# Gates ahead of x on VectorE, o products in pairs, and batch 0's root spread by TensorE, in a fused attention and two-MLP kernel

## The chip, the cores and the metric

One core of a Trainium2 chip runs the whole program. The metric is the device time of one execution in microseconds; the median of three runs of the kernel before is 894.88 us (893.85 to 895.17). TensorE's clock has two levels, 1.2 and 2.4 GHz, and the profile gives the granted one as a share of the higher.

## The reference

Three stages over batch 8, sequence 576, everything in float32:

```
kv  = einsum('bhsd,bhse->bhde', k, v)                    # 8 heads, d = 64
o   = einsum('bhsd,bhde->bhse', q, kv)
x   = o / sqrt(mean(o*o, -1) + 1e-6) * g_norm            # -> (8, 576, 512)

h   = relu(x @ w_in); u, v = h[..., :512], h[..., 512:]
v_n = (v - mean(v)) / sqrt(var(v) + 1e-6)                # over the last axis
gated = u * (einsum('ts,bsd->btd', w_spatial, v_n) + b_spatial[None, :, None])
y   = gated @ w_out

h   = relu(y @ w_in2)                                    # 512 -> 1024
c   = 3-tap convolution of h along the sequence
out = (h * sigmoid(c)) @ w_out2                          # 1024 -> 512
```

## The kernel before

**Numbers.** Large products take float32r operands, each split in a high part (a rounding copy on ScalarE) and a low part (value minus high part, a subtraction); three matmuls (high x high, high x low, low x high) make one product. `w_out @ w_in2` is multiplied once in the prologue into W (`w_product0` for its first half, `w_product` for its second), so the second stage writes only `gated`, through DRAM.

**Stages.** A prologue, up to 61.5 us; a body for each of the 8 batches, up to about 490 us (batches 1 to 6 in a loop, `body`; batch 0 written by itself in `first_body`; the last without work for a next batch); then `body2` for each batch of the third stage.

**The body of batch b** also makes x of batch b+1. On TensorE: k-v product of b+1 (80 matmuls); five v products (four of 128 rows with 12 matmuls of 512 columns, one of the last 64 rows with 8), and between them the four o products of b+1 and the sums of squares, one for each o; four u products (24 matmuls of 288 columns each); four spatial products (28 each). PSUM has eight banks: pairs 0, 1 and 2 (banks 0 to 5) take the u products in the order 0, 1, 2, 0 and the spatial ones in 1, 2, 0, 1; k-v uses bank 5, the sums of squares 4 and 5, o 6 and 7. So the fourth spatial product writes over the first, and waits for the gate that reads it (`s_g`, line 444); the k-v product of the next body waits for two gates (line 452), its v products for three and four (lines 404, 406) and for all four low parts of x (`s_x`, line 399).

**VectorE** (`body`, line 959) runs in this order: a copy of k-v; for each v tile statistics, the low part of the tile before, and normalising; the mean square; the last low part; `inverse_root` (five operations on 128x288); four `x_scale` (o times g times the spread root); four `gate` (spatial PSUM times u). **ScalarE**: relu of v, o_copy, square, high parts, roots, relu of u, and high parts of x (`x_hi`). **GpSimd** makes the low parts of x (`x_lo`, line 292) and the 64 left rows (`x_rows_left`).

**The root r** is in 4 x 4 rows after the sums of squares and must be on 64 partitions per head. `spread_r` on SP writes it to DRAM (4 DMAs), waits, and reads it back broadcast (2 DMAs) into `r_spread`; `x_scale` waits for that. Behind it on SP's queue stand the stores of the gated tiles; ahead of it the loads of k, v and q of batch b+2.

**The prologue.** SP loads two pieces of w_out and w_in2, then k, v, q of batch 0, then the other two pieces and the rest of w_in2, and once w_out is used, the second half of w_in; after the spread of batch 0's root the first half. TensorE: eight weight products, k-v of batch 0, its o products and sums of squares among further weight products, then the four `w_product`, each of which waits for its low part on VectorE (`W_lo`); then the body of batch 0, whose k-v product of batch 1 stands behind two v products. The low parts of the second half of w_in2, of w_in and w_spatial, and x's tiles 0 and 1 are on GpSimd.

## Time and profile before

| | us |
|---|---|
| median of 3 runs | 894.88 |
| profiled execution | 894.39 |
| its span | 892.6 |
| TensorE busy (matmul) | 841.5 (94%) |
| VectorE busy | 456.3 (51%) |
| ScalarE busy | 383.9 (43%) |
| GpSimd busy | 100.5 (11%) |
| mean granted clock | 0.962 |

The profile is of one execution. Busy times are shares of the span, averaged over stages that differ; matmuls are pipelined and their ends are modelled, so that the starts of successive groups give a better length than their busy time. A wait is put down to the semaphore that came last. The chain of waits is followed back from the last instruction. Times of windows and timelines count from the span's start.

### The profile page before, as it was taken

What the parts mean: (1) busy time and instruction counts of PE and PEld (TensorE: products, weight loads), DVE (VectorE), ACT (ScalarE), POOL (GpSimd) and SP (SyncE); (2) the same over time, 40 slices, a digit from 0 to 9 for tenths busy, and PEclk for the clock granted to TensorE, in tenths of its full rate; (3) what the DMA queues carried; (4) which work ended last, traced back from release to release, by engine and by line L of the source; (5) the groups of instructions that cost most, each with busy time, mean ns of one, the idle gap of its engine ahead of it and who ended that gap; (6) DMA issues with size and microseconds to landing.
All of it is one profiled execution on the core that took longest, in us unless ns stands there. A gap on an engine that the chain in (4) does not pass through costs nothing.

```text
span 892.6 us, 15537 instructions
## 1 busy us (share of the span) xinstructions
PE 841.5 (94%) x6038; PEld 743.9 (83%) x6038; DVE 456.3 (51%) x903; ACT 383.9 (43%) x666; POOL 100.5 (11%) x89
## 2 busy tenths in 40 slices
PE   6779799899998989989899999999999999999998
PEld 5456788878788787977889989899998989899996
DVE  2647356364463644536463746528281746538280
ACT  3426234152341533325133746537372736446371
POOL 1453030300203011030305000000000000000000
PEclk9879899899898998989999999999999999999999
DMA  8184341342413424231311101020201102020101
GB/s 301 48 293 143 105 160 55 94 171 54 159 54 109 155 54 159 80 114 60 93 67 44 65 36 66 34 80 1 101 1 57 56 35 65 35 76 0 47 0 59
DMA packets 24869, 75.49 MB, mean 85 GB/s; under 512 B 2434, under 2 KB 2690, under 8 KB 20740
## 3 DMA queue, kind: packets, MB, share of 16 engines
q1 hardware_dynamic: 24692, 75.04, 25.8%
q8 instruction: 21, 0.34, 0.2%
q14 instruction: 12, 0.10, 0.0%
q10 hardware_dynamic: 144, 0.01, 0.0%
HBM read 56.02 MB, written 19.02 MB: 84 GB/s over the span
## 4 chain that ended last, share of the span: by engine, by line
PE 70%; DVE 12%; DMA 7%; issue 5%; ACT 4%; SPq 1%; DVEq 0%; ACTq 0%
PE ps L393 32%; PE ps L566 22%; PE ps L422 9%; DMA r_spread<-r_scratch 5%; PE ps L355 2%; DVE o_x L911 2%; PE ps L372 2%; DVE r L897 2%; DMA kv_raw<-kv_rest_dram 1%; PE ps L508 1%; DMA r_scratch<-r 1%; DVE bn_stats L924 1%; ACT o_x L624 1%; PE ps L385 1%; DVE v_hg_split L950 1%
## 5 line engine op out<-in xcount | busy, mean ns | idle before, releaser
L393 PE MATMUL ps<-x_gated_split,w_product_split 128*128 128x288 f32 x1536 | 204.8, 294 | 0.0
L393 PEld LDWEIGHTS ps<-x_gated_split,w_product_split 128*128 128x128 f32 x1536 | 204.3, 188 | 0.5
L566 PE MATMUL ps<-w_in_split,v_hg_split 128*128 128x512 f32 x832 | 194.6, 389 | 0.0
L566 PEld LDWEIGHTS ps<-w_in_split,v_hg_split 128*128 128x128 f32 x832 | 155.7, 188 | 32.0
L393 PE MATMUL ps<-w_sp_split,v_hg_split 128*128 128x288 f32 x896 | 136.3, 317 | 21.3 <-DVE work L957 21.3
L393 PEld LDWEIGHTS ps<-w_sp_split,v_hg_split 128*128 128x128 f32 x896 | 133.8, 209 | 22.9 <-DVE work L957 22.9
L1053 DVE SCALAR_TENSOR_TENSOR work<-work,const_cols 128x576 f32<-128x576 f32 x64 | 52.4, 819 | 151.6 <-ACT work L815 151.6
L393 PE MATMUL ps<-x_gated_split,w_in_split 128*128 128x288 f32 x768 | 106.1, 298 | 1.1 <-DVE ms L890 0.6
L393 PEld LDWEIGHTS ps<-x_gated_split,w_in_split 128*128 128x128 f32 x768 | 103.7, 190 | 3.8 <-issue 1.8
L422 PE MATMUL ps<-w_in_split,x_gated_split 128*128 128x512 f32 x384 | 97.8, 406 | 6.1 <-issue 6.1
L422 PEld LDWEIGHTS ps<-w_in_split,x_gated_split 128*128 128x128 f32 x384 | 71.7, 192 | 27.2 <-issue 12.3
L292 POOL TENSOR_TENSOR x_gated_split<-o_x,x_gated_split 128x576 fp32r<-128x576 f32 x30 | 49.7, 1685 | 312.5 <-ACT x_gated_split L639 312.5
L810 ACT ACTIVATE work<-ps 128x576 f32<-128x576 f32 x64 | 41.8, 654 | 71.1 <-PE ps L393 59.7
L911 DVE SCALAR_TENSOR_TENSOR o_x<-o_x,const_cols,r_spread 128x576 f32<-128x576 f32 x32 | 33.2, 1101 | 74.6 <-DMA r_spread<-r_scratch 74.6
L846 ACT ACTIVATE o_x<-ps 128x512 f32<-128x512 f32 x32 | 19.1, 598 | 85.0 <-PE ps L566 85.0
L639 ACT ACTIVATE x_gated_split<-o_x 128x576 fp32r<-128x576 f32 x32 | 21.9, 684 | 78.3 <-DVE o_x L911 77.5
L1059 DVE SCALAR_TENSOR_TENSOR work<-work,const_cols 128x576 f32<-128x576 f32 x64 | 52.0, 813 | 0.6
L815 ACT ACTIVATE work<-work,const_cols 128x576 f32<-128x576 f32 x64 | 49.9, 779 | 2.1
L1064 DVE TENSOR_TENSOR work<-work 128x576 f32<-128x576 f32 x64 | 48.1, 751 | 0.3 <-ACT work L820 0.3
L957 DVE TENSOR_TENSOR work<-ps,work 128x576 f32<-128x576 f32 x32 | 22.8, 747 | 47.5 <-PE ps L393 47.5
L924 DVE BATCH_NORM_STATS2 bn_stats<-work 128x6 f32<-128x512 f32 (+1 forms) x40 | 27.7, 692 | 35.0 <-ACT work L651 28.8
L1070 DVE TENSOR_TENSOR v_hg_split<-work,v_hg_split 128x512 fp32r<-128x512 f32 x64 | 43.8, 685 | 0.0
(92 smaller groups left out, 729.1 us busy)
## 6 DMA issues: line engine op xcount, KB each, us to landing
kv_raw<-kv_main_dram SPq DMA_DIRECT2D x8, 2048.0 KB, 8.7
q_raw<-q_T_dram SPq DMA_DIRECT2D x8, 1152.0 KB, 5.1
r_spread<-r_scratch SPq DMA_DIRECT2D x16, 576.0 KB, 6.6
gated_scratch<-work SPq DMA_DIRECT2D x32, 288.0 KB, 2.2
q_raw<-gated_scratch SPq DMA_DIRECT2D x8, 1152.0 KB, 5.7
out_dram<-o_x SPq DMA_DIRECT2D x32, 256.0 KB, 2.0
work<-w_in_dram SPq DMA_DIRECT2D x3, 1024.0 KB, 9.3
kv_raw<-kv_rest_dram SPq DMA_DIRECT2D x8, 256.0 KB, 9.4
```

Of the source, the lines that this page charges most:

```text
L292: pool.tensor_tensor(XG[:, LO, m, :], o_T[:, m, :], XG[:, HI, m, :].bitcast(F32), ALU.subtract).then_inc(s_x, 1)
L393: last = pe.matmul(pair[bank][:, c, :], st, mo[:, c * HALF:(c + 1) * HALF], start=(n == 0), stop=(n == len(steps) - 1))
L422: last = pe.matmul(dst, x, w, start=(n == 0), stop=(n == len(st) - 1))
L566: last = pe.matmul(PS[:, ROW_BANK[i], :], x, wout2[:, w, f, :], start=(f == 0 and n == 0), stop=(f == FT - 1 and n == len(PASSES) - 1))
L810: act.activation(whole(h_sb[f % 3][:, 1:S + 1]), pair[f % 3], ACT.Relu).then_inc(s_hr, 1)
L815: act.activation(t_sb[f % 2], h_sb[f % 3][:, 1:S + 1], ACT.Copy, scale=cols[:, FT + f:FT + f + 1]).then_inc(s_t0, 1)
L911: dve.scalar_tensor_tensor(out=o_T[:, m, :], in0=o_T[:, m, :], scalar=g_col, in1=rB[:, m, :], op0=ALU.mult, op1=ALU.mult).then_inc(s_xm, 1)
L924: dve.bn_stats(stats[0:n, :], v_sb[i % 2][0:n, :]).then_inc(s_vst, 1)
L1053: dve.scalar_tensor_tensor(out=t, in0=h[:, 0:S], scalar=cols[:, f:f + 1], in1=t, op0=ALU.mult, op1=ALU.add).then_inc(s_cv1, 1)
L1059: dve.scalar_tensor_tensor(out=t, in0=h[:, 2:S + 2], scalar=cols[:, 2 * FT + f:2 * FT + f + 1], in1=t, op0=ALU.mult, op1=ALU.add).then_inc ...
L1064: dve.tensor_tensor(p_sb[f % 2], h_sb[f % 3][:, 1:S + 1], p_sb[f % 2], ALU.mult).then_inc(s_mul, 1)
L1070: dve.tensor_tensor(hg[LO][:, f, :], p_sb[f % 2][:, 0:w], hg[HI][:, f, :].bitcast(F32), ALU.subtract).then_inc(s_hlo, 1)
```

## The change

- **VectorE's body:** mean square and inverse root right after the statistics of the last v tile, ahead of the low part of the fourth and of the last tile's normalising; gate 0; four x_scale; gate 1; four low parts of x and the left rows; gates 2 and 3. GpSimd makes no low part of x any more; the left rows' high part is a copy on ScalarE.
- **o products** come in pairs, behind v products 0 and 2, into banks 6/7 and 4/5. The squares of all four tiles lie in one buffer (the one that later takes the spread root), and one sum of 64 matmuls stands behind the last v product. ScalarE's order follows; the last high part of v stands behind the second relu of u.
- **Batch 0** uses the loop's `body`, with the conversions of w_spatial and b_spatial inside, and its k-v product of batch 1 goes first, behind the last x_scale. Its root is spread by TensorE: four times eight small matmuls with a 0/1 matrix (`spread_r`) that GpSimd builds, into PSUM banks 4 to 7, from which `x_scale(0, m)` reads. No DRAM there.
- **Prologue:** another order of loads and of work, w_in2's raw halves in a buffer of their own, their low parts all on VectorE, W_hi(0) behind the root, `inverse_root(0)` ahead of W_lo(1).

```diff
+KV_BANK, SSQ_BANK, R_BANK, O_BANK = 5, 4, 4, [6, 4, 6, 4]
...
+        with ExitStack() as early:
+            w2_early = early.enter_context(nc.sbuf_tensor("w_in2_raw", [P, 2, MT, F1], F32))
+        w2_raw = [w2_early[:, c, :, :] for c in (0, 1)]
...
+        rB = sb("sq_then_r", [P, MT, S])
...
             load_w0(0)
             load_w0(1)
+            load_w0(2)
             load_kv(0)
+            load_w0(3)
             load_q(0)
-            load_w0(2)
-            load_w0(3)
             sp.dma_start(w2_raw[1], w2[:, :, F1:F2]).then_inc(s_w21_in, DMA)
             w = w_in.rearrange("(j p) n -> p j n", p=P)
+            sp.dma_start(wu_raw, w[:, :, 0:F1]).then_inc(s_winu_in, DMA)
             sp.wait_ge(s_woT, MT)
             sp.dma_start(wv_raw, w[:, :, F1:F2]).then_inc(s_win_in, DMA)
-            spread_r(0)
-            sp.wait_ge(s_w2_lo1, MT)
-            sp.dma_start(wu_raw, w[:, :, 0:F1]).then_inc(s_winu_in, DMA)
...
-                pool.wait_ge(s_xhi, (a + 1) * MT)
...
-            for j in range(MT):
...
+                pool.affine_select(out=selT[:, :, :], in_=selT[:, :, :], compare_op=ALU.not_equal, fill=1.0, base=-32 * g,
+                                   pattern=[[-1, MT], [0, D]], channel_multiplier=1).then_inc(s_selT, 1)
...
-            x_lo(0, 0)
-            x_lo(0, 1)
-            x_rows_left(0)
...
-                if m == 0:
+                if m < 2:
                     pe.wait_ge(s_q_in, (a + 1) * DMA)
                     pe.wait_ge(s_kvd0, a + 1)
                     pe.wait_ge(s_kvd1, a + 1)
-                pe.wait_ge(s_oc, a * MT + m)
+                else:
...
+                for m in range(MT):
+                    for g in range(4):
+                        for c in range(CH):
+                            r = slice(c * D, (c + 1) * D)
+                            last = pe.matmul(PS[g * 32:(g + 1) * 32, SSQ_BANK + c, 0:QS], sel[r, m, :],
+                                             rB[r, m, g * QS:(g + 1) * QS], start=(m == 0), stop=(m == MT - 1))
+                last.then_inc(s_ssq, 1)
+
+            def spread_r(m):
+
+                if m == 0:
+                    pe.wait_ge(s_selT, 4)
+                    pe.wait_ge(s_r, 1)
+                else:
+                    pe.wait_ge(s_xm, m)
                 for g in range(4):
+                    r = slice(g * 32, (g + 1) * 32)
                     for c in range(CH):
...
+                        last = pe.matmul(PS[c * D:(c + 1) * D, R_BANK + g, 0:QS], selT[r, m, :], r0[r, c, :], start=True, stop=True)
+                last.then_inc(s_rP, 1)
...
+                    if n == len(st) - 1 and ahead:
+                        if i == 0:
+                            o_ready(b + 1, 1)
+                        if i == 2:
+                            o_ready(b + 1, 3)
+                        if i == FULL:
+                            square_ready(b + 1)
...
+                first = isinstance(b, int) and b == 0
                 if ahead:
-                    pe.wait_ge(s_g, b * MT - 2)
+                    if first:
+                        pe.wait_ge(s_xm, MT)
+                    else:
+                        pe.wait_ge(s_g, b * MT - 2)
                     kv_product(b + 1)
...
+                    if ahead and i in (0, 2):
+                        o_product(b + 1, i)
+                        o_product(b + 1, i + 1)
+                if ahead:
+                    square_sum(b + 1)
+                if first:
+                    pe.wait_ge(s_winu, MT)
                 for m in range(MT):
                     u_product(b, m, ahead)
+                if first:
+                    pe.wait_ge(s_sp_lo, NT)
+                    pe.wait_ge(s_b, 1)
                 for m in range(MT):
                     spatial_product(b, m)
...
+            for j in (0, 1, 2):
                 for i in range(MT):
                     w_product0(j, i)
             pe.wait_ge(s_fill, FILLS)
             kv_product(0)
+            w_product0(3, 0)
+            w_product0(3, 1)
+            o_ready(0, 1)
             o_product(0, 0)
             o_product(0, 1)
...
             w_product0(3, 2)
             w_product0(3, 3)
...
+            o_ready(0, 2)
+            o_product(0, 2)
+            o_ready(0, 3)
+            o_product(0, 3)
+            square_ready(0)
+            square_sum(0)
+            w_product(0)
+            w_product(1)
+            for m in range(MT):
+                spread_r(m)
+                if m < 2:
+                    w_product(2 + m)
             pe.wait_ge(s_win, MT)
 
-            first_body()
+            body(0, True)
...
+                first = isinstance(b, int) and b == 0
                 if ahead:
                     kv_copy(b + 1)
                 for i in range(NT):
                     v_relu(b, i)
-                    if ahead and i < MT:
+                    if ahead and i in (0, 2):
                         o_copy(b + 1, i)
                         square(b + 1, i)
...
+                    if ahead and i == FULL:
+                        root(b + 1)
                     v_root(b, i)
...
+                    if ahead and i in (0, 2):
+                        o_copy(b + 1, i + 1)
+                        square(b + 1, i + 1)
+                    if first:
+                        sp_hi(i)
+                u_relu(b, 0)
+                u_relu(b, 1)
                 v_hi(b, NT - 1)
-                for m in range(MT):
-                    u_relu(b, m)
+                if first:
+                    b_hi()
+                u_relu(b, 2)
+                u_relu(b, 3)
...
+            for m in range(MT):
+                o_copy(0, m)
             w21_hi(0)
             w21_hi(1)
-            W_hi(0)
             root(0)
             w21_hi(2)
             w21_hi(3)
...
+            for n in range(4):
                 W_hi(n)
...
+            W_hi(4)
+            x_hi(0, 0)
+            W_hi(5)
+            x_hi(0, 1)
+            W_hi(6)
+            x_hi(0, 2)
+            x_hi(0, 3)
             W_hi(7)
 
...
+                if isinstance(a, int) and a == 0:
+                    dve.wait_ge(s_rP, m + 1)
+                    o_q = o_T[:, m, :].rearrange("p (g t) -> p g t", g=4)
+                    dve.scalar_tensor_tensor(out=o_q, in0=o_q, scalar=g_col, in1=PS[:, R_BANK:R_BANK + 4, 0:QS],
+                                             op0=ALU.mult, op1=ALU.mult).then_inc(s_xm, 1)
+                    return
...
+                if m == MT - 1:
+                    dve.wait_ge(s_xr0, a + 1)
+                    dve.tensor_tensor(x_rest[:, :, REST:P], o_T[:, :, FULL * P:S], x_rest[:, :, 0:REST].bitcast(F32),
+                                      ALU.subtract).then_inc(s_xr, 1)
 
...
+                    if ahead and i == FULL:
+                        mean_square(b + 1)
+                        inverse_root(b + 1)
                     if i:
                         v_lo(b, i - 1)
                     v_normalise(b, i)
+                v_lo(b, NT - 1)
+                if isinstance(b, int) and b == 0:
...
+                gate(b, 0)
                 if ahead:
-                    mean_square(b + 1)
-                v_lo(b, NT - 1)
-                if ahead:
-                    inverse_root(b + 1)
                     for m in range(MT):
                         x_scale(b + 1, m)
...
+                gate(b, 1)
+                if ahead:
+                    for m in range(MT):
+                        x_lo(b + 1, m)
+                else:
+                    gated_lo(0, 0)
+                    gated_lo(0, 1)
+                gate(b, 2)
+                gate(b, 3)
...
+            for m in range(MT):
+                square(0, m)
+            w21_lo(0)
             mean_square(0)
+            w21_lo(1)
+            w21_lo(2)
+            w21_lo(3)
             W_lo(0)
             inverse_root(0)
-            for n in range(1, 7):
+            for n in (1, 2, 3):
                 W_lo(n)
...
+            x_scale(0, 0)
+            W_lo(4)
+            x_scale(0, 1)
+            x_lo(0, 0)
+            W_lo(5)
+            x_scale(0, 2)
+            x_lo(0, 1)
+            x_scale(0, 3)
+            W_lo(6)
             x_lo(0, 2)
             x_lo(0, 3)
             W_lo(7)
```

## Rows read from the trace of the kernel before

**Rows 1.** Busy time by stretch: start:end, us, each engine's busy us (instructions), PEclk, DMA.
```profile
61.49:121.24 59.75, 53.20 (x442) 45.18 (x442) 31.00 (x68) 23.66 (x43) 21.81 (x20) 0.90 0.43 140
121.24:447.90 326.66, 305.93 (x2642) 264.93 (x2642) 162.34 (x402) 114.53 (x216) 45.88 (x38) 0.94 0.33 105
...
514.43:892.60 378.17, 374.09 (x2209) 339.88 (x2207) 192.90 (x306) 190.00 (x313) 0.00 (x0) 1.00 0.13 44
```

**Rows 2.** Waits, 126 to 448 us: engine, line waited for, us in total, times, longest.
```profile
PE ps L393 <- DVE work L957: 20.7, 6, 4.0
```

**Rows 3.** Chain of waits, two batches' starts and one root: start, us, what.
```profile
340.46 2.48 PE ps L355 x80
342.94 2.97 PE ps L422 x12
345.91 0.65 PE ps L372 x8
...
369.19 1.96 DVE r L897
...
376.49 7.07 DMA r_spread<-r_scratch
...
395.05 2.48 PE ps L355 x80
```

**Rows 4.** Timeline of TensorE in the same batch: start, us, line, operation, [idle before].
```profile
360.53 0.48 PE L385 MATMUL ps<-o_squared,head_select 64*32 64x144 f32 x16
360.94 12.99 PE L393 MATMUL ps<-x_gated_split,w_in_split 128*128 128x288 f32 x96
373.77 11.30 PE L393 MATMUL ps<-w_sp_split,v_hg_split 128*128 128x288 f32 x84
388.45 6.59 PE L393 MATMUL ps<-w_sp_split,v_hg_split 128*128 128x288 f32 x28 [3.38 <-DVE work L957]
```

**Rows 5.** Busy time by stretch, just after the stall.
```profile
388.00:390.00 2.00, 1.55 (x6) 1.55 (x7) 1.73 (x3) 0.45 (x1) 2.00 (x2) 0.50 0.28 106
```

**Rows 6.** Timeline of VectorE in the same batch.
```profile
348.95 0.55 DVE L944 TENSOR_SCALAR work<-work,mean_var,vrs 128x512 f32<-128x512 f32 x1
...
368.47 0.68 DVE L952 TENSOR_TENSOR v_hg_split<-work,v_hg_split 64x512 fp32r<-64x512 f32 x1 [1.55 <-ACT v_hg_split L669]
...
372.50 0.46 DVE L905 TENSOR_TENSOR r<-r,std 128x288 f32<-128x288 f32 x1
383.58 4.15 DVE L911 SCALAR_TENSOR_TENSOR o_x<-o_x,const_cols,r_spread 128x576 f32<-128x576 f32 x4 [10.62 <-DMA r_spread<-r_scratch]
```

**Rows 7.** Timeline of ScalarE in the same batch.
```profile
367.82 0.62 ACT L669 ACTIVATE v_hg_split<-work 64x512 fp32r<-64x512 f32 x1
```

**Rows 8.** One line by itself, ns min/median/max, then groups by line: busy us, mean ns.
```profile
L911 DVE SCALAR_TENSOR_TENSOR o_x<-o_x,const_cols,r_spread x32: 808/817/1985, 54.2 to 440.0; 128x576 f32<-128x576 f32 x32
...
L1064 DVE TENSOR_TENSOR work<-work 128x576 f32<-128x576 f32 x64 | 48.1, 751 | 0.3 <-ACT work L820 0.3
...
L639 ACT ACTIVATE x_gated_split<-o_x 128x576 fp32r<-128x576 f32 x32 | 21.9, 684 | 78.3 <-DVE o_x L911 77.5
...
L916 DVE TENSOR_TENSOR x_gated_split<-o_x,x_gated_split 128x576 fp32r<-128x576 f32 x2 | 3.2, 1614 | 0.0
```

**Rows 9.** Timeline of TensorE in the prologue.
```profile
14.47 3.78 PE L355 MATMUL ps<-kv_raw 128*64 128x64 f32 x80 [2.90 <-DMA kv_raw<-kv_rest_dram]
...
44.55 10.80 PE L508 MATMUL ps<-v_hg_split 128*128 128x512 f32 x36 [2.82 <-DVE w_product_split L1017]
61.49 8.09 PE L422 MATMUL ps<-w_in_split,x_gated_split 128*128 128x512 f32 x24 [6.14 <-issue]
```

**Rows 10.** Timeline of VectorE in the prologue.
```profile
37.14 1.95 DVE L897 RECIPROCAL r<-std 128x288 f32<-128x288 f32 x1
...
42.38 1.52 DVE L905 TENSOR_TENSOR r<-r,std 128x288 f32<-128x288 f32 x1
```

**Rows 11.** Timeline of GpSimd in the prologue.
```profile
40.68 5.77 POOL L310 TENSOR_TENSOR w_in_split<-work,w_in_split 128x512 fp32r<-128x512 f32 x4
```

More of the change, by code:

```diff
@@ L121, in build @@
         rest_sb = SXr[:, 2, :]
[L122 to L124 removed]
+        rB = sb("sq_then_r", [P, MT, S])
         sel = sb("head_select", [P, MT, 32])
+        selT = sb("head_spread", [P, MT, D])
         cols = sb("const_cols", [P, K * FT + 1])
@@ L331, in _ @@
                                        ALU.subtract).then_inc(s_sp_lo, 1)
-            for m in range(MT):
-                x_lo(1, m)
-            x_rows_left(1)
-            with pool.Fori(2, B) as a:
-                for m in range(MT):
-                    x_lo(a, m)
-                x_rows_left(a)
             for f in range(FT):
@@ L513, in _ @@
             for n in range(11):
-                pe.matmul(PS[:, O_BANK, 0:P], sq[:, 0, 0:P], sq[:, 0, 0:P], start=True, stop=True)
-            for j in (0, 1):
+                pe.matmul(PS[:, O_BANK[0], 0:P], SX[:, 0:P], SX[:, 0:P], start=True, stop=True)
+            for j in (0, 1, 2):
                 for i in range(MT):
@@ L685, in body @@
                         v_hi(b, i - 1)
+                    if ahead and i == FULL:
+                        root(b + 1)
                     v_root(b, i)
-                if ahead:
-                    root(b + 1)
+                    if ahead and i in (0, 2):
[5 more added lines that the diff above has]
+                u_relu(b, 1)
                 v_hi(b, NT - 1)
-                for m in range(MT):
-                    u_relu(b, m)
+                if first:
+                    b_hi()
+                u_relu(b, 2)
+                u_relu(b, 3)
                 if ahead:
@@ L757, in _ @@
             act.activation(vsd[:, :], carrier[:, :], ACT.Sqrt)
-            for j in (0, 1):
+            for j in range(MT):
                 woT_hi(j)
@@ L775, in _ @@
             w21_hi(3)
-            for n in (1, 2, 3):
+            for n in range(4):
                 W_hi(n)
@@ L779, in _ @@
                 win_hi(j)
-            for n in (4, 5, 6):
-                W_hi(n)
-            for m in range(MT):
-                x_hi(0, m)
+            W_hi(4)
[5 more added lines that the diff above has]
+            x_hi(0, 3)
             W_hi(7)
-            first_body()
+            body(0, True)
             with act.Fori(1, B - 1) as b:
@@ L895, in inverse_root @@
                 dve.wait_ge(s_std, a + 1)
-                dve.wait_ge(s_rst, a * 4 * DMA)
+                if isinstance(a, int) and a == 1:
+                    dve.wait_ge(s_rP, MT)
+                if not isinstance(a, int):
+                    dve.wait_ge(s_rst, (a - 1) * 4 * DMA)
                 dve.reciprocal(r0[:, :, :], std[:, :, :]).then_inc(s_nr, 1)
@@ L1018, in W_lo @@
                                   ALU.subtract).then_inc(s_W_lo, 1)
-            for j in (0, 1):
+            for j in range(MT):
                 woT_lo(j)
@@ L1042, in _ @@
             W_lo(7)
-            first_body()
+            body(0, True)
             with dve.Fori(1, B - 1) as b:
```

184 lines of the change are left out of this document (30 added, 154 removed).

## The prediction

> **What bounds the kernel now.** I read the view by stretches first [rows 1]. TensorE is busy 53.20 of 59.75 us in the first batch's body, 305.93 of 326.66 us in the next six, and 374.09 of 378.17 us in the last stage, where the granted clock is 1.00. So TensorE is the bound everywhere, and what can be won is its idle time and its slow time ahead of 447.90 us, where the last batch's v products start. The reader is to see that the clock is 0.90 and 0.94 in the two early stretches and 1.00 in the late one.
>
> The waits of the six bodies come next [rows 2]: TensorE waited six times for the gate on VectorE (L957), 20.7 us in total. The chain of waits says what stands ahead of that gate [rows 3]: the reciprocal at 369.19, the spread of the root through DRAM that starts at 376.49 and takes 7.07 us, then the scaling and the gate. TensorE's own timeline of the same batch [rows 4] gives the price: after 3.38 us of idleness the 28 matmuls of the last spatial tile take 6.59 us, where the 84 before them took 11.30, or 3.77 us per 28. The difference, 2.82 us, is the clock: it is 0.50 at 388 to 390 us, the lower of the two levels (1.2 and 2.4 GHz), after the idleness [rows 5]. One stall costs 3.38 + 2.82 = 6.20 us of a period of 395.05 - 340.46 = 54.59 us [rows 3, 4].
>
> Why TensorE waits: the fourth spatial tile overwrites the PSUM pair of the first, so it needs gate 0. VectorE has the four x_scale ahead of all gates, and they wait 10.62 us for the spread [rows 6].
>
> **Change, part 1: gates and x on VectorE in the loop.** I put T = 342.94, where a batch's first v product starts, and lay the new order out from the same rows.
> - TensorE's work is the same, in another order. A v tile takes 2.97 us, an o product 0.65 [rows 3], a square sum 0.41 for 16 matmuls (360.53 to 360.94, rows 4). New order: v0 to 2.97, o0 and o1 to 4.27, v1, v2 to 10.21, o2 and o3 to 11.51, v3 to 14.5, the short v4 (8 matmuls in place of 12) to 16.5, one sum of 4 x 0.41 = 1.64 to 18.1. The u products then start where they do now (360.94 = T+18.0), the spatial ones at 373.77 = T+30.8, one each 3.77.
> - VectorE per v tile: normalising the first ends at 349.50, 3.6 after the tile (345.91) [rows 3, 6]. So v3, ending at T+14.5, is normalised by T+18.3, with 0.2 for the squares ahead of its relu on ScalarE. The remainder tile's add, relu and statistics are an estimate, three passes of 0.7 (L952 has the same 64x512 in 0.68, rows 6) and 0.5 of short ones: T+20.9. The mean square and the root follow, 0.46 each as the pass L905 [rows 6], then the inverse root, 369.19 to 372.96 = 3.77 us [rows 3, 6]: r is ready at about T+25.7 = 368.6, against 372.96 now. It is 4.3 us earlier, because it stands ahead of two low-part and normalising steps.
> - Those steps pay for it: low part of v3 0.7, normalising the rest 1.4, two copies on ScalarE (0.62 each) [rows 7], low part 0.7. The last low part of v ends at T+29.7. The spatial product starts at T+30.8. That is a slack of 1.1 us, where today there are 4.6 (369.15 to 373.77, rows 4, 6). It is the thinnest cover of the loop.
> - The way from r to the first x_scale is 383.58 - 372.96 = 10.62 us [rows 6] and SP has the same things ahead of it, the loads of k, v and q that were issued long before. So x_scale can start at T+36.3. Gate 0 goes at 30.8 + 3.8 = T+34.6 and ends at T+35.5, before the fourth spatial tile, which starts at T+42.1. **The stall is gone with 6.6 us to spare.**
> - What is late next: four x_scale, 0.81 each, to T+39.5; gate 1 (0.75) to T+40.2; four low parts at 0.75 (the nearest row without GpSimd beside it is L1064, 751 ns; rows 8) and the small one to T+43.5; gate 2 to T+44.2. The next k-v product needs gate 1, the next v product all low parts and gate 2, and starts at T+48.4. Slack 4 to 5 us. The other end of the price of a low part is 1614 ns, L916 [rows 8]: four of those end at T+47, still in time. ScalarE has four high parts of 0.68 [rows 8] one behind the other's x_scale, never last.
> - L911's shortest is 808 ns and its longest 1985 [rows 8]; GpSimd's own subtraction waits for the first high part, so it comes beside the last x_scale. With GpSimd out of the loop the long one goes. The Trainium skill, GPSIMD Engine Reference, section Key points, has the two engines share SBUF interfaces, with contention for VectorE instructions with two SBUF inputs. The trace agrees (1985 against 808 ns); by this rule alone the loop gains up to 1.2 us of VectorE time per batch, which lies in slack and gives nothing.
>
> So each of the six transitions from 121.24 to 447.90 loses its stall. The period of rows 3 gives 6.20 us; the last transition (into the batch without a k-v product) is alike, but I take 1 off for the shorter slow stretch that I expect there: 6.2 x 6 - 1 = 36.2 us. From the other side: 20.7 us of waits [rows 2] plus 6 x 2.82 of clock = 37.6.
>
> **Change, part 2: the prologue.** Now the first v product starts at 61.49, after 6.14 us of idleness; k-v of batch 1 comes later [rows 9]. The new order:
> - Loads: one more weight piece (0.5 MB) stands ahead of k and v. The first 3.4 MB were there at 14.4 [rows 9], so it costs at most 14.4 x 0.52 / 3.4 = 2.2 us: k-v product from 15.8 to 16.6 on, and in return eight or twelve matmuls run in what was the 2.90 us of idleness. It takes 2.5 to 3.8 us (3.78 now, slow clock) [rows 9]; end 20.
> - Then, all dependent: 6 weight matmuls at 0.3 us (10.80 / 36, rows 9), two o products 1.3, six matmuls 1.8, o2 and o3 with the copies between (1.3 + 0.7), the square 0.75, the sum 1.64. End 27.6 to 29.6.
> - Mean square and root 0.46 each, two w_in2 conversions and one of the product on ScalarE (3 x 0.62, rows 7), the low part 0.7. First w_product at 31.2 to 33. TensorE is idle 3.5 us there, so it starts at the slow clock.
> - The inverse root now stands ahead of the next three low parts. It takes 3.77 us, or 43.90 - 37.14 = 6.76 as today in this place, where GpSimd works beside it [rows 10, 11]. GpSimd's w_in low parts come at the same point again, so I take 6.76: r at 38 to 40. w_products 1 to 3 at 3.6 us each (10.80 / 3), with the spreads between. A spread is 8 matmuls; the nearest row is 16 in 0.41, so 0.2 to 0.5 us each. This gives 49.5 to 51.5.
> - The last two spreads and x_scale alternate, each waiting for the other: 2 x (0.3 + 0.8) + one low part 0.75 to 1.6: 52 to 54.5. The k-v product of batch 1 (2.5) ends at 54.5 to 57. I take T0 = 55.4 for the first v product, with batch 1's k-v behind it already.
> What is gone is the trip through DRAM (10.62 us in the loop, rows 6), and the low parts on GpSimd. Its price is the wait for the inverse root.
>
> **The first body.** Without stalls it is 54.59 - 6.20 - 2.48 = 45.9 us from v to the next k-v product. Added: five w_spatial conversions on ScalarE inside the chain, GpSimd's low parts beside VectorE (long operations as L916, rows 8), the two bias rows (0.68 each) and their subtraction ahead of the first spatial product, whose cover is only 1.1 us in the loop's order. I estimate a stall of 1 to 3 us, and half clock behind it 0 to 2.8: 4.0 in all. The second k-v product starts at 55.4 + 45.9 + 4.0 = 105.3, against 121.24 [rows 1]. Gain 15.9, between 9 and 22 when all ends fall together.
>
> **Sum.** 36.2 + 15.9 = 52.1 us. The span of 892.6 becomes 840.5; the profiled execution took 894.39, so 842.3. The median of the runs is 0.49 above it: 842.8. I say 843. From 447.90 on, nothing changes: the last stage has the clock at 1.00 and its work is untouched. Removing 0 of TensorE's matmuls and adding 32 small ones is inside these numbers.
>
> **Rivals.**
> - **A, the forecast:** 843, own range 836 to 850.
> - **B, the prologue gives nothing back:** the wait for the inverse root ahead of w_product 1 and the slow clock behind it eat the DRAM trip, and the first body stalls as long as now. For it: VectorE at 6.76 us in that place [rows 10], and 3 waits in a row. Against it: 6.14 us of idleness goes for certain. 36.2 plus 0 to 8: 851 to 859, say 855.
> - **C, a new stall in the loop:** the last low part of v comes later than T+30.8. Slack 1.1 us. If ScalarE or VectorE slip by 3, each of six bodies pays 1.9 and up to 2.8 at half clock: 843 + 6 x 4.7 = 871. For it: VectorE's work is moved ahead of it. Against it: nearly every term is a measured row.
> - **D, slower than before:** the spread comes so late that x_scale holds gate 1, and all low parts wait behind it on VectorE, with TensorE waiting for them at the next v product. The place is the first v product, its slack 4 to 5 us; beyond that each us costs one per body and the clock 2.8 more. To use up 52 us over six bodies takes 8.7 each, so the way from r to x_scale must be 10.6 + 4.5 + 5.9 = 21 us or more. That is twice the measured value, and I see nothing that would do it. From there on it is over 895, say 905.
> - **E, it doesn't do what it says:** gate 0 still late, stall unchanged, prologue alone gains: 879.
>
> **How the numbers follow.** A 0.68, B 0.15, C 0.11, D 0.03, E 0.03. The time is A's. The range holds A and most of B: 833 to 859; what is outside is C, D, E and a small tail, about 0.2. About 0.2% (1.8 us) is what a measurement of this kernel can tell from no change. Faster: A, B, C and E, 0.97 less 0.01 that I leave to no change; slower: D, 0.03.
>
> **What would show it.** The wait of TensorE for L957's gate inside the loop goes from 20.7 us to about zero, the period between two k-v products from 54.6 to 48.4, the clock to 1.00 there. r_spread lands some 6 us before gate 2. The first v product comes at 55, behind a k-v product. If C holds, the fresh wait is the first spatial product on the low part of v; if B, the second k-v product starts at 113 or later. The forecast is wrong if the period is over 49.5 us, or if that product starts outside 99 to 112.

## The result, and the profile after

The changed kernel takes 832.76 us (median of 4 runs, 832.22 to 833.83), beside 895.02 us of the kernel before on the same chip (893.85 to 896.32): ratio 0.9306, interval 0.9289 to 0.9322. The forecast was 843.0, with a range from 833 to 859; the time is 0.24 us below its lower end. The profiled span is 830.7 us, against 892.6. TensorE is busy 98% of it and not 94%. In experiments 7 and 10 one execution of four took far longer than the others (1610.06 and 2818.20 us); it is left out of their medians and ranges.

The view by stretches, with the columns of [rows 1]: the first body, the six transitions of the loop, the last batch's body, the last stage, and one period (from one k-v product to the next).

```profile
56.60:103.78 47.18, 45.14 (x365) 40.01 (x364) 30.69 (x72) 23.70 (x44) 7.13 (x5) 1.00 0.38 120
103.78:386.06 282.28, 282.28 (x2641) 253.87 (x2642) 172.41 (x432) 116.74 (x222) 0.00 (x0) 1.00 0.38 121
386.06:452.58 66.52, 65.99 (x458) 63.56 (x457) 40.38 (x93) 34.71 (x57) 12.21 (x8) 1.00 0.17 59
452.58:830.70 378.12, 374.08 (x2209) 339.97 (x2207) 192.98 (x306) 190.04 (x313) 0.00 (x0) 1.00 0.13 44
150.80:197.85 47.05, 47.05 (x442) 42.29 (x444) 28.73 (x72) 19.45 (x37) 0.00 (x0) 1.00 0.39 126
```

The loop's TensorE has no idle time at all, at full clock. Set against [rows 1], the 61.9 us split so:

| | before | after | gain | predicted |
|---|---|---|---|---|
| start to the second k-v product | 121.24 | 103.78 | 17.46 | 15.9 |
| to the last batch's first v product | 326.66 | 282.28 | 44.38 | 36.2 |
| the rest | 444.70 | 444.64 | 0.06 | 0 |

The waits of TensorE in the whole run. The 20.7 us of L957's gate [rows 2] are gone, and what is left lies ahead of 90 us, but for 0.53 us in the last batch's body, at 402.48. The five longest:

```profile
PE ps L486 <- DVE w_product_split L986: 5.9, 2, 3.5
PE ps L364 <- DVE sq_then_r L848: 1.7, 1, 1.7
PE ps L336 <- DMA kv_raw<-kv_rest_dram: 1.7, 1, 1.7
PE ps L385 <- DVE w_sp_split L947: 1.3, 1, 1.3
PE ps L385 <- ACT work L636: 1.3, 2, 0.7
```

TensorE in one batch of the loop. Beside [rows 4], the spatial products run as one block of 112, where the last 28 alone took 6.59 us behind 3.38 of waiting.

```profile
153.21 3.01 PE L416 MATMUL ps<-w_in_split,x_gated_split 128*128 128x512 f32 x12
156.16 1.20 PE L352 MATMUL ps<-q_raw,kv_double 64*64 64x288 f32 x16
157.28 5.73 PE L416 MATMUL ps<-w_in_split,x_gated_split 128*128 128x512 f32 x24
...
166.93 1.97 PE L416 MATMUL ps<-w_in_split,rest_split 128*128 128x512 f32 x8
168.84 1.24 PE L364 MATMUL ps<-sq_then_r,head_select 64*32 64x144 f32 x64
170.00 12.99 PE L385 MATMUL ps<-x_gated_split,w_in_split 128*128 128x288 f32 x96
182.83 15.02 PE L385 MATMUL ps<-w_sp_split,v_hg_split 128*128 128x288 f32 x112
```

VectorE in the same batch, the answer to [rows 6]: the last low part of v is done at 181.87, 0.96 us ahead of the spatial product (1.1 predicted); gate 0 goes at 186.82, before x_scale and not behind it.

```profile
177.64 0.46 DVE L870 TENSOR_TENSOR r<-r,std 128x288 f32<-128x288 f32 x1
...
181.18 0.69 DVE L926 TENSOR_TENSOR v_hg_split<-work,v_hg_split 64x512 fp32r<-64x512 f32 x1 [1.22 <-ACT v_hg_split L649]
186.82 0.76 DVE L931 TENSOR_TENSOR work<-ps,work 128x576 f32<-128x576 f32 x1 [4.95 <-PE ps L385]
188.72 3.01 DVE L881 SCALAR_TENSOR_TENSOR o_x<-o_x,const_cols,sq_then_r 128x576 f32<-128x576 f32 x4 [1.15 <-DMA sq_then_r<-r_scratch]
191.65 0.75 DVE L931 TENSOR_TENSOR work<-ps,work 128x576 f32<-128x576 f32 x1
192.31 2.75 DVE L886 TENSOR_TENSOR x_gated_split<-o_x,x_gated_split 128x576 fp32r<-128x576 f32 x4
```

TensorE between the root and the first body, the answer to the end of [rows 9]:

```profile
30.66 5.25 PE L486 MATMUL ps<-v_hg_split 128*128 128x512 f32 x12 [3.52 <-DVE w_product_split L986]
...
51.07 0.51 PE L378 MATMUL ps<-r,head_spread 32*64 32x144 f32 x16 [0.98 <-DVE o_x L876]
52.60 4.08 PE L336 MATMUL ps<-kv_raw 128*64 128x64 f32 x80 [1.02 <-issue]
56.60 3.02 PE L416 MATMUL ps<-w_in_split,x_gated_split 128*128 128x512 f32 x12
```

### The profile page after: what moved, and what is told of

It is laid out like the page before. It is cut to its first block, busy times and chain, and to the rows that moved or that the text cites. A ratio compares the mean times of both kernels' runs of the same rounds, so it can differ in the third digit from the quotient of the medians.

```text
span 830.7 us, 15568 instructions
## 1 busy us (share of the span) xinstructions
PE 811.2 (98%) x6102; PEld 731.3 (88%) x6102; DVE 467.2 (56%) x945; ACT 386.5 (47%) x674; POOL 39.0 (5%) x44
## 4 chain that ended last, share of the span: by engine, by line
PE 91%; DVE 5%; DMA 1%; ACT 1%; issue 1%; SPq 0%; ACTq 0%
PE ps L385 49%; PE ps L545 24%; PE ps L416 11%; PE ps L336 3%; PE ps L352 2%; DMA kv_raw<-kv_rest_dram 1%; PE ps L486 1%; PE ps L364 1%; DVE bn_stats L898 1%; DVE r L862 0%; DVE work L918 0%; DVE v_hg_split L924 0%; DVE vrs L916 0%; PE ps L474 0%; DVE r L870 0%
## 5 line engine op out<-in xcount | busy, mean ns | idle before, releaser
L385 PE MATMUL ps<-w_sp_split,v_hg_split 128*128 128x288 f32 x896 | 120.2, 295 | 1.3 <-DVE w_sp_split L947 1.3
L385 PEld LDWEIGHTS ps<-w_sp_split,v_hg_split 128*128 128x128 f32 x896 | 119.2, 188 | 1.5 <-issue 1.5
L385 PE MATMUL ps<-x_gated_split,w_in_split 128*128 128x288 f32 x768 | 104.4, 296 | 1.3 <-ACT work L636 1.3
L416 PE MATMUL ps<-w_in_split,x_gated_split 128*128 128x512 f32 x384 | 93.4, 397 | 0.0
L778 ACT ACTIVATE work<-work,const_cols 128x576 f32<-128x576 f32 x64 | 49.9, 779 | 2.1
L898 DVE BATCH_NORM_STATS2 bn_stats<-work 128x6 f32<-128x512 f32 (+1 forms) x40 | 27.7, 691 | 35.9 <-ACT work L631 29.6
L783 ACT ACTIVATE work<-work 128x576 f32<-128x576 f32 x64 | 42.9, 670 | 0.0
L631 ACT ACTIVATE work<-ps 128x512 f32<-128x512 f32 x32 | 19.1, 597 | 33.8 <-PE ps L416 33.5
```

What stands on the lines that cost most here:

```text
L385: last = pe.matmul(pair[bank][:, c, :], st, mo[:, c * HALF:(c + 1) * HALF], start=(n == 0), stop=(n == len(steps) - 1))
L416: last = pe.matmul(dst, x, w, start=(n == 0), stop=(n == len(st) - 1))
L778: act.activation(t_sb[f % 2], h_sb[f % 3][:, 1:S + 1], ACT.Copy, scale=cols[:, FT + f:FT + f + 1]).then_inc(s_t0, 1)
L783: act.activation(p_sb[f % 2], t_sb[f % 2], ACT.Sigmoid).then_inc(s_sig, 1)
L898: dve.bn_stats(stats[0:n, :], v_sb[i % 2][0:n, :]).then_inc(s_vst, 1)
```

## The experiments

My theory after the result: the stall went as forecast, and the 8.2 us that the loop is shorter than forecast are TensorE's own, from how the small matmuls are grouped. I call a group of small-tile matmuls (64\*64 or 64\*32, the o products and the sums of squares) between full ones (128\*128) a visit. The rivals are that the waits inside the v products cost, or that more idle time went than I had counted. For the prologue I had claims on the DRAM trip and on GpSimd's load.

**1. Gate 0 alone** (e1_gate0_first). The kernel before, with one line moved, in the loop (shown) and in the first body:

```
                     inverse_root(b + 1)
+                gate(b, 0)
+                if ahead:
                     for m in range(MT):
                         x_scale(b + 1, m)
-                for m in range(MT):
+                for m in range(1, MT):
```

> The kernel before with one edit: gate 0 ahead of the four x_scale, in the loop and in the first body. My theory: the order of gate 0 alone removes the stall and the slow clock behind it. Six transitions at 6.2 us less about 1, plus the short one of the first body (0.55 idle, some 0.8 in all): 895.0 - 37 = 858 us, period between two k-v products in the loop 48.4. Rival: gate 0 alone isn't enough, because the spread lands as late as before (T+40.6) and the low parts on GpSimd end 8 us behind it, at T+49 to T+52, past the next v product at T+48.4: then a new wait of 1 to 3 us on GpSimd's low parts at the first v product, and half clock behind it, so 865 to 880 us and a period of 50 to 53.

Measured: 865.81 us (865.69 to 866.86), ratio 0.9679 (0.9657 to 0.9700). The spatial block is unbroken. But x is late now, in TensorE's timeline and in its waits:

```profile
319.55 3.00 PE L422 MATMUL ps<-w_in_split,x_gated_split 128*128 128x512 f32 x12 [0.67 <-POOL x_gated_split L292]
...
350.42 15.02 PE L393 MATMUL ps<-w_sp_split,v_hg_split 128*128 128x288 f32 x112
```

```profile
PE ps L422 <- POOL x_gated_split L292: 6.5, 6, 2.7
```

The six transitions take 297.92 us and not 326.66: 28.7 us are this one move. In this order GpSimd's low parts are what the next batch waits for. The time is at the low end of the rival's; the period, 49.2 us (316.33 to 365.57), lies between the theory's 48.4 and the rival's 50.

**2 and 3. One o product a visit** (e2_single_o_two_waits, e3_single_o_four_waits). The kernel after, with o products and their copies and squares one behind each v product again; the first keeps the two waits for free o banks, the second has a wait at each of four.

```
-                    if ahead and i in (0, 2):
+                    if ahead and i < MT:
                         o_product(b + 1, i)
-                        o_product(b + 1, i + 1)
```

> The changed kernel with one o product behind each of v products 0 to 3 in place of pairs behind 0 and 2 (ScalarE's copies and squares follow); the two semaphore waits stay where they are. Visit theory: each break of a run of full-array matmuls by small ones costs some 0.4 to 0.45 us (before: v tile 2.97 beside an o product 0.65; after: two v tiles 5.66, a pair 1.13), so two more visits in each of seven bodies cost 7 x 0.9 = 6 us: 839 us, loop period 47.05 to 47.9. Wait theory: the cost was in the waits ahead of the last matmul of a v product, and as these stay two, the time stays at 832.8 and the period at 47.05.

> As the one with single o products, and with a wait ahead of the last matmul of each of v products 0 to 3 too, as the kernel before has them. Visit theory: no different from the run with two waits, 839 us and a period of 47.9. Wait theory: here the 6 us appear, 839, while the run with two waits stays at 832.8. If both count, this one lies over the other: each wait some 0.1 to 0.3 us, so up to 843.

Measured: 838.34 us (837.38 to 839.27), ratio 0.9371 (0.9349 to 0.9394), and 837.98 us, ratio 0.9369 (0.9348 to 0.9391). The period is 47.88 us in both, 0.83 above the kernel after. TensorE of the first of them:

```profile
154.16 3.01 PE L416 MATMUL ps<-w_in_split,x_gated_split 128*128 128x512 f32 x12
157.10 0.72 PE L352 MATMUL ps<-q_raw,kv_double 64*64 64x288 f32 x8
157.75 3.03 PE L416 MATMUL ps<-w_in_split,x_gated_split 128*128 128x512 f32 x12
```

From one start to the next, a v product is 2.94 us and an o product 0.65 again, where the kernel after has 5.67 for two and 1.13 for two. The period has two visits more and the same 442 matmuls, and takes 0.41 us more for each; waits that are already fulfilled cost nothing.

**4. The sum in two visits** (e4_sum_two_visits). The kernel after, with the sums of three tiles behind the fourth v product and that of the last behind the fifth. The wait for the squares moves with them, from the fifth v product into the fourth (not shown).

```
+                    if ahead and i == FULL - 1:
+                        square_sum(b + 1, (0, 1, 2))
                 if ahead:
-                    square_sum(b + 1)
+                    square_sum(b + 1, (3,))
```

> The changed kernel with the sum of squares in two visits: three tiles (48 matmuls) behind v product 3, the last (16) behind v product 4; one wait, ahead of v product 3's last matmul. Visit theory: one more visit in each of seven bodies, 0.4 to 0.45 us each, 3 us in all: 836 us, period 47.5. Theory that the saving of the sum lay in its length alone (64 matmuls in 1.17 us in place of 4 x 0.41): less than 0.15 us per body, 833 to 834 us. The wait may add up to 0.3 per body if the fourth square is not ready at v product 3's end.

Measured: 837.43 us (834.73 to 838.91), ratio 0.9352 (0.9323 to 0.9380); period 47.86, 0.81 longer. One visit more costs as much as two did above, but it brought a wait along:

```profile
165.53 2.79 PE L417 MATMUL ps<-w_in_split,x_gated_split 128*128 128x512 f32 x11
168.47 0.50 PE L417 MATMUL ps<-w_in_split,x_gated_split 128*128 128x512 f32 x1 [0.15 <-ACT sq_then_r L610]
168.90 0.99 PE L364 MATMUL ps<-sq_then_r,head_select 64*32 64x144 f32 x48
169.82 2.10 PE L417 MATMUL ps<-w_in_split,rest_split 128*128 128x512 f32 x8
```

The v product with the wait inside takes 3.37 us to the start of the sum (165.53 to 168.90), where one with small matmuls behind it takes 2.96 in experiment 2: 0.41 us, of which 0.15 show as idle time. The other 0.40 us are those of the visit. So grouping is shown as the cause; that the price is 0.4 us here too is read from this one trace.

**5. Low parts of x back on GpSimd** (e8_x_lo_gpsimd), in the order of the kernel after.

```
+            for m in range(MT):
+                x_lo(1, m)                    # GpSimd
+            with pool.Fori(2, B) as a:
+                for m in range(MT):
+                    x_lo(a, m)
...
-                if ahead:
-                    for m in range(MT):       # VectorE
-                        x_lo(b + 1, m)
```

> The changed kernel with the low parts of x of batches 1 to 7 back on GpSimd (the left rows too); gate order, pairs and the single sum stay. My prediction costed the move to VectorE at nothing: the spread lands 4 to 5 us earlier than before, so four low parts on GpSimd from T+37 at 1.64 us and the left rows end at T+44.5, ahead of the next v product at T+47: 832.8 us, period 47.05, no wait of TensorE. Rival, from the run with gate 0 alone: there GpSimd's low parts held the first v product in every body by 0.7 to 0.8 us and by 2.7 in the last. If the margin here is used up by VectorE instructions slowed beside GpSimd (1.96 us for the last x_scale) and the gates behind them, the period is 47.5 to 48.5 and the time 836 to 842 us.

Measured: 832.06 us (829.37 to 833.86), ratio 0.9282 (0.9247 to 0.9318), period 47.05, no wait of TensorE in the loop. GpSimd has them from 189.85 to 197.15 and the v product starts at 199.57. In this order the engine makes no difference. In experiment 1 GpSimd was late: r (the inverse root) there comes as in the kernel before, 372.96 - 342.94 = 30.0 us behind the first v product [rows 3, 6], and not 24.9. That the earlier r is the whole reason was not tried by itself.

**6. GpSimd held back** (e5_gpsimd_after_root). The kernel after with one wait, so that GpSimd's low parts of w_in start behind batch 0's inverse root:

```
+            pool.wait_ge(s_r, 1)
             for j in range(MT):
                 pool.wait_ge(s_win_hi, j + 1)
```

> The changed kernel with one wait more: GpSimd starts the low parts of w_in only when batch 0's root is ready. Theory contention: the inverse root of batch 0 took 7.1 us on VectorE (30.52 to 37.65) because GpSimd works beside it from 31.74 on, against 3.8 in the loop; alone it takes 3.8, r is ready at 34.3, w_product(1) can start at 35.9 where w_product(0) ends (38.31 now), with no idleness of 2.40 us ahead of it and so no half clock in it (4.60 us now, 2.95 the next): the first v product 3 to 4 us earlier, 829 us. Rival: the durations are VectorE's own in that place (the operations are slow for another reason), r stays at 37.6: 832.8 us, or later if GpSimd's work, 13.7 us from 34.3 on, now falls on x_scale and the low parts of x: 834.

Measured: 828.42 us (826.74 to 828.96), ratio 0.9246 (0.9218 to 0.9273). The inverse root on VectorE, first in the kernel after, then with GpSimd silent:

```profile
30.52 1.95 DVE L862 RECIPROCAL r<-std 128x288 f32<-128x288 f32 x1
32.49 0.83 DVE L864 TENSOR_TENSOR std<-r 128x288 f32<-128x288 f32 x1
33.36 1.42 DVE L866 TENSOR_TENSOR std<-std,ms 128x288 f32<-128x288 f32 x1
34.82 1.28 DVE L868 TENSOR_SCALAR std<-std 128x288 f32<-128x288 f32 x1
36.13 1.52 DVE L870 TENSOR_TENSOR r<-r,std 128x288 f32<-128x288 f32 x1
```

```profile
29.29 1.94 DVE L863 RECIPROCAL r<-std 128x288 f32<-128x288 f32 x1
31.27 0.46 DVE L865 TENSOR_TENSOR std<-r 128x288 f32<-128x288 f32 x1
31.76 0.46 DVE L867 TENSOR_TENSOR std<-std,ms 128x288 f32<-128x288 f32 x1
32.25 0.31 DVE L869 TENSOR_SCALAR std<-std 128x288 f32<-128x288 f32 x1
32.60 0.46 DVE L871 TENSOR_TENSOR r<-r,std 128x288 f32<-128x288 f32 x1
```

3.77 us and not 7.13. From the first `w_product` to the second k-v product it is 68.57 us and not 73.05. The time, too, is where the theory put it.

**7 and 8. Batch 0's root through DRAM** (e6_root0_dram, e7_root0_dram_gpsimd_after), in the kernel after: once alone, once with GpSimd held back. With it the four x_scale stand together behind `W_lo(5)`, and the k-v product of batch 1 has no wait ahead of it.

```
-            for m in range(MT):
-                spread_r(m)                   # TensorE
-                if m < 2:
-                    w_product(2 + m)
+            w_product(2)
+            w_product(3)
...
+            spread_r(0)                       # SP, through DRAM
```

> The changed kernel with batch 0's root spread through DRAM as in the kernel before, in the new order of work (w_products run through, the four x_scale behind W_lo(5), k-v product of batch 1 without its wait). My prediction counted the DRAM trip's going as the prologue's gain. If so, this run gives it back: 4 to 8 us, 837 to 841 us. Rival: on TensorE's path four spreads and four x_scale alternate (43.5 to 52.5 us), while the trip takes 10.6 us from r at 37.65, beside w_products 1 to 3: spread there at 48.3, x_scale to 51.3, low parts to 54.3, first v product at 54.5 in place of 56.6, and the k-v product at full clock: 830 to 831 us. Then TensorE's spreading was not what made the prologue shorter.

> Both: root of batch 0 through DRAM, and GpSimd's low parts of w_in only behind that root. If contention and the DRAM rival hold: r at 34.3, spread at 45, the first v product at 51.5 to 53, 827 to 829 us. If only one holds, the time of that run. If neither, over 836 us.

Measured: 830.68 us (829.05 to 830.78), ratio 0.9260 (0.9223 to 0.9296); and 831.20 us (830.42 to 832.38), ratio 0.9272 (0.9244 to 0.9299), where 827 to 829 was expected. The landing of the first k-v load moves by some 2 us between executions, so the traces, one of each kernel, are compared from the first `w_product` to the second k-v product:

| | spread by TensorE | through DRAM |
|---|---|---|
| GpSimd free | 73.05 | 71.58 |
| GpSimd held | 68.57 | 70.50 |

With GpSimd beside VectorE the trip through DRAM is 1.5 us better than TensorE's spread; with GpSimd held it is 1.9 worse. The latter is not the trip's own length: from r to the first x_scale it is 10.19 us in both. But GpSimd, held back, now works beside x_scale, from 44.60 to 50.81, and the four take 5.22 us and not 3.01:

```profile
46.93 5.22 DVE L868 SCALAR_TENSOR_TENSOR o_x<-o_x,const_cols,sq_then_r 128x576 f32<-128x576 f32 x4 [4.47 <-DMA sq_then_r<-r_scratch]
44.60 6.21 POOL L312 TENSOR_TENSOR w_in_split<-work,w_in_split 128x512 fp32r<-128x512 f32 x4
```

With GpSimd free, the trip leaves TensorE idle for 4.34 us ahead of the first v product:

```profile
46.46 2.55 PE L337 MATMUL ps<-kv_raw 128*64 128x64 f32 x80
53.35 4.61 PE L417 MATMUL ps<-w_in_split,x_gated_split 128*128 128x512 f32 x12 [4.34 <-DVE x_gated_split L872]
```

**9 and 10. What waits is moved** (e9_bias_early, e10_prologue_order). First the kernel of experiment 6 with `b_hi` ahead of the last high part of v, and the bias subtraction ahead of its low part, in the first body. Then also this in the prologue:

```
             w_product(1)
-            for m in range(MT):
+            w_product(2)
+            spread_r(0)
+            w_product(3)
+            for m in range(1, MT):
                 spread_r(m)
-                if m < 2:
-                    w_product(2 + m)
```

and the low parts `W_lo(0)` to `W_lo(3)` ahead of `inverse_root(0)` on VectorE, with the mean square behind the first of them, and `W_hi(0)` ahead of the root on ScalarE.

> The kernel after, with GpSimd's low parts of w_in held back until batch 0's inverse root is done (as in e5_gpsimd_after_root, 828.4 us) and, in the first body only, the reduction of b taken ahead of the last high part of v on ScalarE, and the subtraction of the bias ahead of the last low part of v on VectorE. In the kernel after, TensorE waits 1.30 us at 88.70 for VectorE's subtraction (L947). Theory 'that wait is an order of work, not a lack of it': it goes, about 827.1. Rival 'what is late next is the last low part of v itself': the wait moves to the first spatial product and stays at 0.7 to 1.3 us, 828 to 828.5.

> The kernel of e9_bias_early, with the high and low parts of block 0 of batch 0's weights taken earlier, and TensorE's order changed to w_product 2, spread of r 0, w_product 3, spreads of r 1 to 3, so that the last w_product waits for no spread. Theory 'the prologue behind the root still has idle TensorE between the products and the spreads, and what waits can be moved': up to 4 us less than e9, about 823 to 824. Rival 'each further change between spreads and products costs a visit, and r comes 1.9 us later because VectorE makes the low parts ahead of it': within 0.5 us of e9, or 1 to 2 us slower.

Measured: 826.47 us (826.27 to 828.05), ratio 0.9267 (0.9201 to 0.9334); and 824.49 us (824.40 to 825.55), ratio 0.9246 (0.9161 to 0.9331). The kernel before spread from 885.8 to 896.8 us on this chip, hence the wide intervals. In the first, the wait of 1.30 us ahead of the spatial product is gone and none has come in its place; from the first `w_product` to the second k-v product it is 67.38 us, where experiment 6 had 68.57. In the second, from the sum of squares to the second k-v product it is 69.7 us and not 72.1 (the k-v product of batch 0 started 0.46 later there, and the medians differ by 1.98), but the last spreads stand in a row and each waits for x_scale:

```profile
40.40 0.50 PE L379 MATMUL ps<-r,head_spread 32*64 32x144 f32 x16
41.88 0.51 PE L379 MATMUL ps<-r,head_spread 32*64 32x144 f32 x16 [0.97 <-DVE o_x L879]
44.19 0.51 PE L379 MATMUL ps<-r,head_spread 32*64 32x144 f32 x16 [1.81 <-DVE o_x L879]
```

**11. The first body of the kernel before in another order** (e11_first_body_early_o), its o products and sums behind the v products, the k-v product of batch 1 behind the first of them, and ScalarE's copies and squares one v tile earlier; the other bodies are untouched.

```
                     v_product(b, i, ahead)
...
+                    if first:
+                        if i:
+                            o_product(1, i - 1)
+                        if i > 1:
+                            square_sum(1, i - 2)
```

> The kernel before, with batch 0's body alone in another order: its four o products and squares' sums stand behind the v products and not among the u products, and the k-v product of batch 1 behind the first v product. The root of batch 1 is thus ready long before the body ends. All other bodies and the DRAM route stay. In the kernel before, this body takes 57.3 us, with a wait of 4.29 us for ScalarE's squares (L629) and three of 0.6 to 0.7; the kernel after has 47.2. Theory 'what the change gained in this body is those waits, and the slow clock behind them': 4 to 8 us less, 887 to 891. Rival 'the body is as long because its clock is slow after the prologue, whatever its order': within 1 us of 895.

Measured: 891.25 us (887.58 to 895.91, 10 runs), ratio 0.9985 (0.9950 to 1.0020): inconclusive, and my edit missed its aim. The wait for the fourth square is still there:

```profile
89.64 0.73 PE L385 MATMUL ps<-o_squared,head_select 64*32 64x144 f32 x16 [4.74 <-ACT o_squared L644]
```

ScalarE's program still had the fourth o copy behind the last v tile's relu, which waits for VectorE. So the square came at 88.91, behind a wait of 2.20 us on ScalarE, and TensorE's order could not bring it forward.

**12. The stall filled** (e12_filled_stall). The kernel before with 26 matmuls more, into a free bank, where TensorE waits for gate 0.

```
                 for m in range(MT):
+                    if ahead and m == 3:
+                        for n in range(26):
+                            pe.matmul(PS[:, 6, 0:HALF], vn[:, HI, 0, 0:P], wsp[:, HI, 0, 0:HALF], start=True, stop=True)
                     spatial_product(b, m)
```

> The kernel before, with 26 further matmuls into a free bank ahead of the fourth spatial product of bodies 1 to 6, in the stretch in which TensorE waited for gate 0 (L957) and its clock fell to 0.50. Extra work only; the outputs do not depend on it. In the kernel before, the spatial product behind the wait took 6.59 us for 28 matmuls, where the one of 84 took 11.30. Theory 'the wait cost twice, once as idle time and once through the clock that fell in it, and busy TensorE keeps the clock': period 54.4 to about 51.5, 876 to 880 us. Rival 'the product behind the wait is slow for what it reads or writes': its time stays 6.6 us, and the kernel takes 895 to 905.

Measured: 880.74 us (880.13 to 883.35), ratio 0.9880 (0.9808 to 0.9952); 14.5 us less, with more work; 876 to 880 was expected.

```profile
363.11 11.30 PE L393 MATMUL ps<-w_sp_split,v_hg_split 128*128 128x288 f32 x84
374.25 3.59 PE L466 MATMUL ps<-w_sp_split,v_hg_split 128*128 128x288 f32 x26
377.94 3.98 PE L393 MATMUL ps<-w_sp_split,v_hg_split 128*128 128x288 f32 x28
```

The place of the stall is as long as it was (3.59 us of matmuls beside 3.38 idle), the granted clock behind it (377.90 to 382.00) is 1.00 and not 0.50 [rows 5], and the product there takes 3.98 us and not 6.59 [rows 4]. Five periods, 121.19 to 381.92, are 52.15 us each, where the kernel before has 54.76: 2.61 less, which is 6.59 - 3.98. So the price of the clock behind the stall is shown apart from the idle time.

## Why the prediction was right or wrong

- **The stall of the loop: right, in mechanism and size.** Experiment 1 shows that gate 0's place made it, experiment 12 what the clock had in it. Without the 8.1 us of the next point the loop gained 36.3 us; the step said 36.2.
- **The step that failed: "TensorE's work is the same, in another order."** I laid the new order out with 2.97 us for a v tile, 0.65 for an o product and 0.41 for a sum, prices that [rows 3, 4] show for groups broken up by others. In the new groups two v tiles take 5.67 (not 5.94), two o products 1.13 (not 1.30), v3 and v4 together 4.76 (not 5.0), and 64 matmuls of the sum 1.16 (not 1.64). The period without a stall is 47.05 and not 48.4: 1.35 us by 6 bodies is 8.1 us, a term I had at nothing, and four fifths of what the forecast was too long. Experiments 2 and 3 show 0.83 of the 1.35, the two visits fewer for o products, by undoing them; the 0.48 of the sum is read from the trace.
- **Orders and slacks in the loop: right.** From the first v product on, r was forecast at 25.7 us and came at 24.9, x_scale 36.3 and 35.5, gate 0 34.6 and 33.6, the spatial product 30.8 and 29.6. All were 0.8 to 1.2 us early; the sum of squares had ended 1.3 early. Rival C's wait, with a slack of 0.96 us, did not occur, and rival D's neither.
- **The prologue and the first body: total near (17.46, 15.9 forecast), in part by luck.** The prologue came out 1.2 us longer than forecast and the first body 2.7 shorter. In the prologue one reason was wrong too. First v product at 56.6 (55.4 forecast), first `w_product` at 30.66 (31.2 to 33), inverse root 7.13 (6.76). I wrote that "what is gone is the trip through DRAM" and put its 10.62 us beside the change. Experiment 7 shows that with the trip put back the time is no longer than with four spreads (830.68 and 832.76 us); in experiment 8 it is longer, by less than what GpSimd costs x_scale there. What the prologue gained came from the order around it, and by how much each move of it gained is not tried apart. A spread is 16 matmuls in the trace and not 8; its 0.43 us lie within my 0.2 to 0.5.
- **The first body: 47.2 us, where 49.9 was forecast.** The stalls and the slow clock that I put at 4.0 us are some 2.6 against the loop's 44.6 from v to the next k-v product, 2.04 of them waits (0.74 and 1.30); the other 1.35 is the grouping again. Against the 57.3 before, less the k-v product, the traces give 4.5 us of waits less, 2 of slow clock in the v products and 1.7 in the u products, and 1.35 of grouping. That is a reading: experiment 11, meant to show it, did not remove the wait.
- **Low parts on VectorE give nothing: right** in this order (experiment 5). Behind gate 0 alone TensorE waited 6.5 us for GpSimd's (experiment 1); whether the move would have saved them there was not run.
- **Rivals B and E** fell by the second k-v product at 103.8, not 113 or later, and by a loop without waits.

Together: +8.2 in the loop and +1.6 ahead of it, 9.8 us of the 10.2 that the forecast was too long.

The version of experiment 10 has the lowest time, 824.5 us, and is faster than experiment 9's on the same chip. How far it is below the kernel after is not settled: they ran on different chips, and the intervals of their ratios overlap.

## What to carry to other kernels

A bound engine's program is not a bag of matmuls with fixed prices: count how often it goes from one shape to the other, and take prices from a row with the same neighbours. A stall on TensorE can cost its idle time and the slow clock behind it; fill it, if it can't go. Before replacing a transfer, see what the other engines do in that place. Keep GpSimd silent beside VectorE's chain on the critical path, and look where its work goes instead.

## What the runs showed of the hardware

- One visit of small-tile matmuls more between full ones, with the same matmuls in all, cost 0.41 us (experiments 2 and 3) and 0.40 (experiment 4, its wait set aside). A wait inside a product that showed as 0.15 us idle cost 0.41 (experiment 4).
- 3.38 us idle on TensorE were followed by a granted clock of 0.50, and 28 matmuls took 6.59 us; with 26 matmuls in that place they took 3.98 at 1.00 (experiment 12).
- GpSimd's work on 128x512 tiles beside VectorE's on 128x288: 0.46 us becomes 0.83 to 1.52, and the one-input TENSOR_SCALAR 0.31 becomes 1.28, while RECIPROCAL stays at 1.95, though GpSimd ran beside only the last 0.73 us of it (experiment 6). In the kernel before, a 0.46 us operation at 39.12 kept its time with GpSimd at work from 37.70 on, so not every one is lengthened. The Trainium skill, GPSIMD Engine Reference, section Key points, puts the contention at VectorE instructions with two SBUF inputs or in a 2-port mode. The measured rows agree as to RECIPROCAL and, but for that one, the two-input ones; that the TENSOR_SCALAR runs in such a mode is not shown here.
- An x_scale that reads the root from PSUM took 0.81 us at 43.53 with GpSimd's L310 running beside it until 45.33; the four that read it from SBUF took 5.22 us in experiment 8, where GpSimd was active, and 3.01 in experiment 7, where it had ended.
